# Expert stage of a 3,072-token MoE kernel: relu's rows turned by a DRAM round trip and VectorE's 32x32 transposes from tile 3 on, second product one tile later

## The reference, cut to what matters

```python
logits = x @ w_gate                       # x: 3072 tokens of 512 features, 8 experts
e_idx = np.argmax(logits, axis=1)
gate_w = softmax(logits)[arange(N), e_idx]
eom = 1.0 / (1.0 + np.exp(-(x @ w_output_gate)))
for e in range(E):
    mask = e_idx == e
    h = np.maximum(x[mask] @ w1[e], 0.0)  # w1[e]: 512 x 1024
    ye = h @ w2[e]                        # w2[e]: 1024 x 512
    out[mask] = gate_w[mask, None] * eom[mask, e, None] * ye
```

## Time and profile before

| what | value |
|---|---|
| median of 3 runs | 763.2 us (761.56 to 763.55) |
| profiled execution, its own time | 763.58 us |
| its span, first to last instruction | 761.9 us |
| mean granted clock of TensorE | 0.994 |
| PE busy | 733.5 us, 96% |
| DVE / ACT / POOL busy | 446.5 / 307.2 / 182.4 us |
| DMA | 85.02 MB, mean 112 GB/s |
| stage C in the loop | from about 450 us to the end |

### The profile page before, as it was taken

One profiled execution on the slowest core, in us unless ns is written; L12 is line 12 of the kernel. 1 busy time (PEld: TensorE's weight loads), 2 busy tenths in 40 slices (PEclk: granted clock), 3 DMA queues, 4 the chain that ended last, 5 costly groups with the idle time before them and its releaser, 6 DMA issues.

```text
span 761.9 us, 16533 instructions
## 1 busy us (share of the span) xinstructions
PE 733.5 (96%) x5480; PEld 638.8 (84%) x5481; DVE 446.5 (59%) x753; ACT 307.2 (40%) x467; POOL 182.4 (24%) x352
## 2 busy tenths in 40 slices
PE   2899999999999999999989999999999999999995
PEld 2698998999899989998978788888888888888883
DVE  5677787878676766777826736224645454544311
ACT  3543444344434443443325445234444444454221
POOL 2121544354211211121121312212121222212121
PEclk9999999999999999999999999999999999999998
DMA  9713334432322232222016434310526261601000
GB/s 328 245 56 113 99 99 143 147 97 97 112 95 69 69 122 86 69 69 84 15 43 249 173 137 166 130 42 31 215 81 237 67 247 62 228 23 55 13 28 21
DMA packets 22922, 85.02 MB, mean 112 GB/s; under 512 B 3950, under 2 KB 4334, under 8 KB 20976
## 3 DMA queue, kind: packets, MB, share of 16 engines
q1 hardware_dynamic: 16080, 64.82, 24.2%
q0 software_dynamic: 5952, 16.98, 7.0%
q10 hardware_dynamic: 864, 2.88, 1.1%
HBM read 73.78 MB, written 14.09 MB: 115 GB/s over the span
## 4 chain that ended last, share of the span: by engine, by line
PE 95%; DVE 2%; DMA 1%; issue 1%; ACT 0%; DVEq 0%; POOLq 0%; SPq 0%; ACTq 0%
PE banks L1136 77%; PE banks L1167 4%; PE banks L1292 3%; PE banks L1157 3%; PE banks L1189 3%; PE banks L1149 2%; PE banks L1269 2%; DMA q_sb<-q_t 1%; DVE he L834 0%; DVE prob L819 0%; PE banks L1219 0%; DVE ys L1104 0%; DVE ssum L815 0%; DVE uT_lo L823 0%; ACT e_sb L616 0%
## 5 line engine op out<-in xcount | busy, mean ns | idle before, releaser
L1136 PE MATMUL banks<-slots_hi_lo,rT_hi 128*128 128x512 f32 x464 | 146.0, 396 | 0.4 <-DVE rT_lo L991 0.4
L1136 PE MATMUL banks<-slots_hi_lo,xsT_hi 128*128 128x512 f32 x464 | 124.5, 390 | 0.3 <-issue 0.3
L987 DVE TENSOR_TENSOR xsT_lo<-banks,xsT_hi 128x512 fp32r<-128x512 f32 x30 | 20.8, 692 | 149.0 <-ACT xsT_hi L662 149.0
L1136 PEld LDWEIGHTS banks<-slots_hi_lo,xsT_hi 128*128 128x128 f32 x464 | 86.7, 188 | 18.9 <-issue 1.0
L1136 PEld LDWEIGHTS banks<-slots_hi_lo,rT_hi 128*128 128x128 f32 x464 | 84.9, 188 | 17.0 <-DVE rT_lo L991 0.8
L1136 PE MATMUL banks<-slots_hi_lo,rT_lo 128*128 128x512 f32 x232 | 90.8, 391 | 0.0
L553 POOL DMA_INDIRECT out<-ys,rows_out x29 | 30.2, 1041 | 238.1 <-DVE ys L1104 231.5
L1136 PE MATMUL banks<-wout_hi,uT_hi 128*128 128x264 f32 x384 | 83.1, 298 | 2.0 <-DVE uT_lo L823 2.0
L1096 DVE TENSOR_TENSOR slots_hi_lo<-raw_w,slots_hi_lo 128x1024 fp32r<-128x1024 f32 x56 | 64.9, 1220 | 27.3 <-ACT slots_hi_lo L743 27.3
L1136 PE MATMUL banks<-wout_hi,uT_lo 128*128 128x264 f32 x384 | 78.6, 286 | 0.0
L1136 PE MATMUL banks<-wout_lo,uT_hi 128*128 128x264 f32 x384 | 78.4, 286 | 0.0
(11 more groups left out here) (162 smaller groups left out, 1204.4 us busy)
## 6 DMA issues: line engine op xcount, KB each, us to landing
raw_w<-experts SPq DMA_DIRECT2D x14, 2048.0 KB
v_sb<-v_win SPq DMA_DIRECT2D x24, 384.0 KB, 4.7
k_sb<-k_win SPq DMA_DIRECT2D x22, 384.0 KB, 3.6
x_rows<-x SPq DMA_DIRECT2D x24, 264.0 KB, 2.1
q_sb<-q_t SPq DMA_DIRECT2D x24, 256.0 KB, 2.7
stage<-experts POOLq DMA_DIRECT2D x8, 512.0 KB, 5.5
weights<-w_both ACTq DMA_DIRECT2D x4, 512.0 KB, 9.4
weights<-w_both SPq DMA_DIRECT2D x4, 512.0 KB, 12.8
```

Source lines behind the costliest of these rows:

```text
L987: nc.vector.tensor_tensor(xsT_lo[:, :], xs_ps, xsT_hi[:, :].bitcast(F32), ALU.subtract).then_inc(xtlo_s, 1)
L1136: ins = mm(o, lhs, rhs(part, k, n), start=(k == first and lhs is not None and part == 0 and parts == (0, 1)), stop=(k == final and parts = ...
```

## The change

From tile 3 on (`BY_PE = 3`) PE no longer turns relu's rows. ACT stores `r_sb` into a DRAM tensor `r_rows` of 4 x 128 x 256 (`store_r`) and loads it again as `r_quads`, 128 partitions of 4 KB: partition 32a + j holds quarter a of the rows 4j to 4j + 3 (`load_r`). DVE then transposes `r_quads` in blocks of 32x32 into `r_turned` (`turn_r`), and the high and low parts are made from there. The order of the hidden units over the partitions that comes out of this differs from before; the host lays out w2 in the same order (`quad_rows`).

Since the round trip is longer, the second product comes one tile later: PE's step is hidden(t), xs_turn(t + 1), expert_out(t - 2). DVE and ACT make the parts of tile t - 1 in step t, and result, gate value and scatter move back by a tile. Tiles 0 to 2 still go through PE, and tile 2's second product is spread over the steps 3 (5 chunks) and 4 (3 chunks). Behind the loop two products stand for PE instead of one. ACT waits for the product of tile t - 2 before it overwrites a w2 slot. A few tensors move in SBUF (`ys_odd` to the common region, the stage region by 4 KB).

The diff, without the declarations of semaphores, the argument `r_dram` and the moved SBUF addresses:

```diff
 SKIP = NTOK + 7 * P
 EARLY = NBLK - 3
 GW = 32
+QUADS = P // 32
+BY_PE = 3
+LEAST = 6
 C_ID, C_IOTA, C_PART, C_SEL, C_END = 0, P, P + NTILE, P + NTILE + 1, P + NTILE + 1 + 2 * E
 C_TRI, C_MASK = 0, P
 C_IOTA_BF = C_MASK + POS * KEYS
...
         r_sb = rc.take("r_sb", [P, DF], F32)
         rT_hi += [rc.take("rT_hi1", [P, DF], F32R)]
         rT_lo += [rc.take("rT_lo1", [P, DF], F32R)]
-        ys = [rc.take(f"ys{n}", [P, DM], F32) for n in range(2)]
+        r_quads = rc.take("r_quads", [P, DF], F32)
+        r_turned = rc.take("r_turned", [P, DF], F32)
+        ys = [rc.take("ys_even", [P, DM], F32), ys_odd]
+        assert rc.at <= stage_at
         banks = ctx.enter_context(nc.psum_tensor("banks", [P, 8 * BANK], F32))
...
                 step(At(n, 1))
             step(At(0, NBLK - 2))
+        def by_pe(t):
+
+            return isinstance(t.i, int) and t.i < BY_PE
+
         def last_tile(eng):
             eng.wait_ge(tbl_s, 2)
-            return eng.value_load(expert_tbl[0:1, 2, 0:1], min_val=E - 1, max_val=NTILE - 1)
+            return eng.value_load(expert_tbl[0:1, 2, 0:1], min_val=E - 1 - LEAST, max_val=NTILE - 1 - LEAST)
         def walk_c(eng, last, step, final=None, begin=2):
             def live(t):
-                with eng.If(last >= t.i):
+                with eng.If(last >= (t + -LEAST).i):
                     step(t)
-            for t in range(begin, 4):
+            for t in range(begin, 6):
                 step(At(0, t))
-            with eng.Fori(2, NTILE // 2) as n:
+            with eng.Fori(3, NTILE // 2) as n:
                 live(At(n, 0))
                 live(At(n, 1))
             if final:
                 with eng.If(last % 2 == 0):
-                    final(At(last // 2, 0))
+                    final(At(last // 2 + LEAST // 2, 0))
                 with eng.Else():
-                    final(At(last // 2, 1))
+                    final(At(last // 2 + LEAST // 2, 1))
         def by_slot(eng, e, emit):
...
             with eng.If(tile_info(eng, 1, t) == 1):
                 pieces(0, tile_info(eng, 0, t) + 1)
             with eng.If(tile_info(eng, 1, t + -1) == 1):
+                if eng is nc.scalar:
+                    eng.wait_ge(out_ps_s, t.i - 1)
                 pieces(1, tile_info(eng, 0, t + -1) + 1)
...
             def step(t):
                 gather(t + 2)
+                if by_pe(t):
+                    scatter(t + -1)
+                elif not by_pe(t + -1):
+                    scatter(t + -2)
+
+            def ending(t):
                 scatter(t + -1)
+                scatter(t)
             last = last_tile(pool)
             step(At(0, 1))
-            walk_c(pool, last, step, scatter)
+            walk_c(pool, last, step, ending)
         @block.scalar
...
             def relu(t):
                 act.wait_ge(hid_s, t.i + 1)
-                at_least(act, rt_ps_s, t.i)
-                nc.scalar.activation(r_sb[:, :], h_ps, ACT.Relu).then_inc(relu_s, 1)
+                if by_pe(t + -1):
+                    at_least(act, rt_ps_s, t.i)
+                else:
+                    act.wait_ge(r_store_s, (t.i - BY_PE) * 16)
+                if by_pe(t):
+                    nc.scalar.activation(r_sb[:, :].rearrange("p (k a i) -> p a k i", a=QUADS, k=KF),
+                                         h_ps.rearrange("p (a k i) -> p a k i", a=QUADS, k=KF), ACT.Relu).then_inc(relu_s, 1)
+                else:
+                    nc.scalar.activation(r_sb[:, :], h_ps, ACT.Relu).then_inc(relu_s, 1)
+
+            def store_r(t):
+
+                act.wait_ge(relu_s, t.i + 1)
+                at_least(act, r_load_s, (t.i - BY_PE) * 16)
+                act.dma_start(r_dram.rearrange("a p n -> p a n"),
+                              r_sb[:, :].rearrange("p (a n) -> p a n", a=QUADS)).then_inc(r_store_s, 16)
+
+            def load_r(t):
+
+                act.wait_ge(r_store_s, (t.i - (BY_PE - 1)) * 16)
+                at_least(act, r_turn_s, t.i - BY_PE)
+                act.dma_start(r_quads[:, :],
+                              r_dram.rearrange("a (j b) n -> (a j) (b n)", b=QUADS)).then_inc(r_load_s, 16)
             def high_r(t):
-                act.wait_ge(rt_ps_s, t.i + 1)
                 at_least(act, out_ps_s, t.i - 1)
-                nc.scalar.activation(rT_hi[t.par][:, :], turn_ps, ACT.Copy).then_inc(rthi_s, 1)
+                if by_pe(t):
+                    act.wait_ge(rt_ps_s, t.i + 1)
+                    nc.scalar.activation(rT_hi[t.par][:, :], turn_ps, ACT.Copy).then_inc(rthi_s, 1)
+                else:
+                    act.wait_ge(r_turn_s, t.i - (BY_PE - 1))
+                    nc.scalar.activation(rT_hi[t.par][:, :], r_turned[:, :], ACT.Copy).then_inc(rthi_s, 1)
             def load_k(b):
                 act.dma_start(k_sb[b][:, :, :, :].rearrange("p a c n -> p (a c n)"), k_in[b, :, :]).then_inc(load_s[b], 16)
...
             def step_c(t):
                 relu(t)
+                if not by_pe(t):
+                    store_r(t)
                 xt(t + 1)
-                high_r(t)
+                if by_pe(t):
+                    high_r(t)
                 gate_exp(t + 1)
+                if not by_pe(t):
+                    load_r(t)
+                    if not by_pe(t + -1):
+                        high_r(t + -1)
                 if isinstance(t.i, int) and t.i == 2:
                     pieces(1, 1)
                 split_next(act, pieces, t)
-            walk_c(act, last, step_c)
+            walk_c(act, last, step_c, high_r)
         @block.vector
...
                 dve.wait_ge(xthi_s, t.i + 1)
                 nc.vector.tensor_tensor(xsT_lo[:, :], xs_ps, xsT_hi[:, :].bitcast(F32), ALU.subtract).then_inc(xtlo_s, 1)
+            def turn_r(t):
+
+                dve.wait_ge(r_load_s, (t.i - (BY_PE - 1)) * 16)
+                dve.wait_ge(rthi_s, t.i)
+                nc.vector.transpose(r_turned[:, :].rearrange("p (c j b) -> p b c j", c=KF, b=QUADS),
+                                    r_quads[:, :].rearrange("p (b c i) -> p b c i", b=QUADS, c=KF)).then_inc(r_turn_s, 1)
+
             def low_r(t):
                 dve.wait_ge(rthi_s, t.i + 1)
-                nc.vector.tensor_tensor(rT_lo[t.par][:, :], turn_ps, rT_hi[t.par][:, :].bitcast(F32),
-                                        ALU.subtract).then_inc(rtlo_s, 1)
+                nc.vector.tensor_tensor(rT_lo[t.par][:, :], turn_ps if by_pe(t) else r_turned[:, :],
+                                        rT_hi[t.par][:, :].bitcast(F32), ALU.subtract).then_inc(rtlo_s, 1)
             dve.wait_ge(mask_in_s, 16)
             softmax_a(At(0, 0))
...
             V.tensor_copy(expert_tbl[:, 0, 0:NTILE], t32["e"][:, :])
             V.memset(expert_tbl[:, 0, NTILE:], E - 1)
-            V.tensor_scalar(expert_tbl[:, 2, 0:1], ne["end"][:, E - 1:E], -1.0, None, ALU.add)
+            V.tensor_scalar(expert_tbl[:, 2, 0:1], ne["end"][:, E - 1:E], -1.0 - LEAST, None, ALU.add)
             V.tensor_tensor(expert_tbl[:, 1, 0:NTILE], t32["new"][:, :], t32["more"][:, :], ALU.mult).then_inc(tbl_s, 1)
             gate_value(At(0, 0))
...
             def step_c(t):
                 xt(t + 1)
                 gate_max(t + 1)
-                low_r(t)
-                result(t + -1)
-                gate_value(t + 1)
+                if by_pe(t):
+                    low_r(t)
+                    result(t + -1)
+                    gate_value(t + 1)
+                elif not by_pe(t + -1):
+                    turn_r(t + -1)
+                    low_r(t + -1)
+                    result(t + -2)
+                    gate_value(t)
                 if isinstance(t.i, int) and t.i == 2:
                     pieces(1, 1)
                 split_next(dve, pieces, t)
-            walk_c(dve, last, step_c, result)
+            def ending(t):
+                turn_r(t)
+                low_r(t)
+                result(t + -1)
+                result(t)
+
+            walk_c(dve, last, step_c, ending)
         @block.tensor
...
             def step_c(t):
                 hidden(t, range(KD))
-                expert_out(t + -1, range(0, 5))
                 xs_turn(t + 1)
-                r_turn(t)
-                expert_out(t + -1, range(5, KF))
-
-
-            walk_c(pe, last_t, step_c, lambda t: expert_out(t, e=E - 1), begin=3)
+                if by_pe(t + -1):
+                    expert_out(t + -1, range(0, 5))
+                elif by_pe(t + -2):
+                    expert_out(t + -2, range(5, KF))
+                else:
+                    expert_out(t + -2)
+
+            def ending(t):
+                expert_out(t + -1)
+                expert_out(t, e=E - 1)
+
+            walk_c(pe, last_t, step_c, ending, begin=3)
 def kernel(q, k, v, mem_k, mem_v, moe_w_in, moe_w_out, moe_g_ln, moe2_w_gate, moe2_w_output_gate, moe2_w1, moe2_w2):
...
     w_both = np.concatenate([rows(moe_w_in, KD), rows(moe_w_out, KF)], axis=1)
     wout_t = rows(moe_w_out.T, KD)
```

(8 more changed lines are left out.)

11 lines of the change are left out of this document (8 added, 3 removed).

## The result

The changed kernel takes 771.0 us (median of 4 runs, 768.5 to 772.3) against 762.4 us for the kernel before on the same chip (4 runs, 761.4 to 763.6): a ratio of 1.011, 95% interval 1.007 to 1.014. It is slower by 1.1%, where 750 us was forecast. The profiled execution took 769.8 us, with a span of 768.1.

The account below looks back on a forecast made before the run. PE, busy 96% of the span, was taken as the bound: 22.7 us of removed turns, less 3.0 at the change of mode, 4.5 at the end and 1.7 of clock, gives 13.5, so 763.6 becomes 750 us; range 744 to 765.

Parts of the forecast that it names:

- the pair's margin: Two successive weight-splitting tiles: the tile after starts VectorE's xt at T+4.56 against 4.95 allowed, 0.4 us spare, no steady-state stall.
- the term for turn_r: VectorE's 32x32 transpose of the reloaded rows: 1.15 us taken, between bounds of 0.81 and 2.45.
- rival 2: VectorE's transpose takes two passes, 2.45 us, stalling PE after weight-splitting tiles: 766 us, up to 778; chance 0.18.
- the store's landing (T+4.1): ScalarE's 512 KB store to DRAM lands 2.9 us after issue, at T+4.1; T is the start of a tile's relu.
- its data has until the next tile's turn_r (T+14): DRAM load of relu's rows, issued to T+4.55 after relu's start T: even 5.5 us of landing is covered.
- the change of mode: Switch from PE turning to the round trip: stalls of 0.7, 0.6 and 1.7 us at xt of tiles 5 to 7, sum 3.0.
- Rival 3: Weights' 2 MB load collides with the round trip, hurting only if a store is caught: 765 us; chance 0.05.
- rival 1: DRAM store of relu's rows lands in 4.2 us, using up the spare in weight-splitting tiles: 757 us; chance 0.15.
- The end: After the loop's dead tiles the last transpose comes late: PE stalls 4.9 us against 0.4 before, net 4.5.
- The clock: PE's clock drops to the lower level after the 4.9 us stall at the end, losing 1.7 us.
- the beat of 11.38: PE's time per plain tile: forecast 12.24 less 0.87 for the removed turns, 11.37 us.
- the chain of a pair: VectorE from one xt to the next across two weight-splitting tiles: 13.1 us, 1.73 more than PE's time per tile.

Follow-up runs that it names:

- run 9: Changed kernel with the transpose's output written without gaps (token groups misordered, output wrong); single run: 760.0 us beside 762.0 for the kernel before.
- run 2: Changed kernel with a plain VectorE copy in place of the transpose, same strides, rows not turned: 760.2 us, ratio 0.998.
- run 3: Changed kernel with two DRAM buffers, so store_r no longer waits for the previous tile's load: 764.7 us, ratio 1.004.
- run 6: Changed kernel storing and loading only 32 of 256 columns (64 KB each way, turned rows incomplete): 769.9 us, ratio 1.010.
- run 13: Changed kernel with turn_r writing runs of 32 neighbouring elements and xt reading tokens in permuted order, result right: 759.8 us, ratio 0.998.
- run 14: Kernel before with the second product one tile later, PE still turning rows, right behind xs_turn: 762.9 us, ratio 1.002.
- run 5: Changed kernel with VectorE's four register reads of the expert table moved behind turn_r: 753.7 us, ratio 0.990.
- run 15: Changed kernel with two DRAM buffers, reads behind turn_r, high_r before load_r, VectorE's and ScalarE's ending inside the loop, contiguous transpose output: 743.1 us, ratio 0.975.
- run 1: Second product one tile later in the changed step order, PE still turning rows at the step's end, no round trip: 784.0 us, ratio 1.027.

## Why the forecast was wrong

**The step that failed is the pair's margin, and in it the term for turn_r.** 1.15 us was taken; the runs show 1.99. The prediction named it as the number that would overturn the forecast, and named the stride of four elements; run 9 shows that this stride is the cause (1.23 without it), and runs 2 and 9 that the length is worth some 11 us. Rival 2 was right in kind: waits in each of the five later pairs, 1.3 to 2.4 us, and the clock falls behind two of them. But 771 came at 1.99 us, where rival 2 still left a small gain. Its prices for a longer transpose count from the store's landing (T+4.1), though the list above it has high_r behind load_r (T+4.6). By its own list, with turn_r from T+3.0, the first tile is late only from 1.6 us of transpose on and the second from 1.15. So the margin lasts to 1.54 us, not 1.3; the stall is 0.9 us a pair at 1.99 us, and 1.8 in place of 2.35 at 2.45 us. The measured waits are larger. Two reasons show in the timelines: the start of the chain (the next step), and the handoff. Where PE waited for xsT_lo in the pairs, it started 0.28 to 0.42 us after that pass had ended (617.69 + 0.68 = 618.37, and PE at 618.79); the forecast left 0.05, from T+5.65 to T+5.7. That takes most of the 0.4 us of margin before anything is late.

Being nearer to one row than to the bound was no safe way to choose: the copy with the same strides takes 1.07 us in all, the transpose 0.75 us more than without them, and no row of before could show that. The estimate from "VectorE: DVE Perf Modes" in the Trainium skill, section "The three transpose paths", 2.5 us, was closer to the result than mine. For the contiguous form it is twice too long (1.23). For that form the one element per cycle and lane of "Vector Engine (DVE) Microarchitecture Reference" in the Trainium skill, section 3.8, agrees with the trace, where a pass with two inputs over 1024 columns (rT_lo) takes 1.23 us too. The strided form (1.99) doesn't follow from it.

**A second step failed by itself: "its data has until the next tile's turn_r (T+14)".** The load's first reader in time is not turn_r. It is store_r of the next tile, at T+12.5, as both share one buffer in DRAM, and xt stands behind that store. With 2 MB of weights beside it the load took 6 us in a pair (583.42 to 589.55) and 10 at the change of mode. Rival 3 saw the collision and looked at turn_r only. Run 3 gives the store's wait 6 us, run 6 1 us.

The first tile's timeline in run 13 shows how the margin goes even where the transpose is short. high_r starts 2.0 us late, by two parts: the store leaves 0.9 us late, behind that load, and it lands in 4.0 us where 2.9 was taken. The second part is rival 1's mechanism (a store landing in 4.2 us). Over all tiles high_r waits for the store's landing 13 times in run 2 (19.7 us) and 7 times in run 13 (11.2 us), and once in the changed kernel, where the long transpose ends later than the landing. No run shortened the landing alone, so its price is open.

In run 13 the 10 us missing from the forecast are 5.2 us more of PE's waits (13.1 on VectorE's parts and on issue, against 3.0 + 4.9) and 3.4 more of clock (three falls of 1.7 us, behind the waits at 448, 733 and 742 us, against one). That these waits come from the late store, its landing, the handoff and the change of mode is read from the timelines; it isn't split up by runs. Whether two DRAM buffers with the contiguous output and nothing else would give 750 wasn't run.

**The change of mode** was forecast as 3.0 us of stalls in tiles 5 to 7. It is one wait of 3.4 us at tile 5, of the second cause, and then 3.4 us of clock, for which the sum had nothing. With two buffers the forecast's picture appears in kind: waits of 2.3 and 1.7 us at tiles 6 and 7.

**The end** was 4.9 us in one stall. It came as two, 2.6 and 2.5 us. The late turn_r behind the dead tiles was right (VectorE idle 5.0 us), but the product of tile 27 needs its rT_lo right behind that of tile 26, and it is late as well. The forecast's own list has that part ready at T+6.8 and PE free at T+5.7, a stall of 1.1 us that it left out; the sum stays 4.9, as PE then ends later and waits less for tile 28. Sum and clock loss (1.7) fit: 5.1 + 1.7 against 4.9 + 1.7.

**The clock** in steady state was left out of the forecast's sum (rival 2 had it). Three places at 1.7 us and one at 3.4: 8.5 us in all, of which 1.7 was in the sum (the end).

**Right:** 208 turns and 22.7 us off PE; the beat of 11.38; 13.1 us for the chain of a pair (run 13, with 1.23 us for the transpose in place of 1.15); median landings of 3.3 and 3.6 us inside the bounds of 2.1 and 5.5 (2.9 taken for the store); the move of the product costs little (1.4 us, run 14). An eighth of the bytes gains 1 us (run 6). The register reads, 2.95 us, sat in the chain of the pair in plain view; that moving them is worth 17 us was not asked.

**Open:** of the 14.6 us between the spans of the changed kernel and run 5 (768.1 and 753.5), 9.7 are waits of PE in the view of waits (19.9 and 10.2) and 3.4 are clock (8.5 and 5.1 by the stretches); 1.5 stays unassigned. The times of run 5 also scatter more, 751.0 to 759.3 us, than those of run 15, 741.8 to 743.9; why was not tried. The difference between runs 3 and 6 stays open too.

## What to carry to other kernels

Before work is moved off the bounding engine, write down the chain of its most loaded tile on the engine that takes it, register reads and queue waits included. A forecast with 0.4 us of margin is a forecast of whatever the least known term says, and the first thing to do is to make margin (here by reading registers where the engine waits anyway). For every buffer of a round trip ask who writes it next, not only who reads it, and what is queued behind that writer.

## What the runs showed of the hardware that I had not expected

- A 32x32 transpose of 128x1024 fp32 takes 1.23 us with an output in runs of 32 or more neighbouring elements and 1.99 us with an output stride of 16 bytes; a plain copy with the same stride takes 1.07 us.
- A 512 KB load issued 1.8 us after 2 MB of weights landed almost 10 us after its issue, against 3.6 in the median.
- The clock fell to its lower level (1.2 GHz, 0.50 granted) behind PE's waits of 3.39, 2.38, 2.36 and 2.63 us, at 448.8, 618.8, 693.9 and 743.9 us. It stayed at 1.00 behind those of 1.76 and 2.03 us, at 545 and 582, and behind one of 2.48 at 753.7. In run 3 it fell behind one of 1.85 us, at 545.6. The length of the wait alone doesn't tell.
- In the second tile of a pair three register reads and the branches stood on VectorE's path, 2.7 us; with the reads where the engine waits for another one, 0.55 us were left (run 5). On PE, with eight short matmuls at the end of a step, the next step started 0.5 us late, and such waits were 9.4 us in 15 places; with the turns ahead of a long product they were 1.3 us (runs 1 and 14).
